# Attention with softmax reciprocals read from the transposed tile, the output product in two halves, and everything behind the scores one step later

## What is computed

```python
scores = scale * np.matmul(q, k.transpose(0, 1, 3, 2))
cum = np.cumsum(np.maximum(s, 0.0), axis=-1)
bias = -(cum[:, :, :, None] - cum[:, :, None, :])
scores = np.where(causal, -1000000000.0, scores + np.minimum(bias, 0.0))
attn = np.exp(scores - np.max(scores, axis=-1, keepdims=True))
attn = attn / (np.sum(attn, axis=-1, keepdims=True) + 1e-09)
attn_out = np.matmul(attn, v)
x = xn(attn_out) ; h = silu(x @ w_gate) * (x @ w_val) ; y = h @ w_out     # xn: RMS norm
h = y @ w_in ; out = (h - np.tanh(h)) @ moe2_w_out
```

## Time and profile before

| what | value |
|---|---|
| three runs, median | 1107.66 us (1103.31 to 1108.92) |
| the profiled execution | 1106.37 us |
| its span, first to last instruction | 1104.6 us |
| mean granted clock of PE | 0.997 |
| busy: PE, DVE, ACT, POOL | 1065.3, 431.2, 421.1, 172.2 us |

### The profile page before, as it was taken

One profiled execution on the slowest core, in us unless ns is written; L12 is line 12 of the kernel. 1 busy time (PEld: TensorE's weight loads), 2 busy tenths in 40 slices (PEclk: granted clock), 3 DMA queues, 4 the chain that ended last, 5 costly groups with the idle time before them and its releaser, 6 DMA issues.

```text
span 1104.6 us, 18165 instructions
## 1 busy us (share of the span) xinstructions
PE 1065.3 (96%) x6516; PEld 980.2 (89%) x6516; DVE 431.2 (39%) x1203; ACT 421.1 (38%) x1030; POOL 172.2 (16%) x184
## 2 busy tenths in 40 slices
PE   5888998899999999999999999999999999999998
PEld 4767777689999999999999999999999999999997
DVE  6656666654432222322322333533223232332322
ACT  5666677663431232222222233533223232322322
POOL 8767777640000000000000000000000000000000
PEclk9999999999999999999999999999999999999999
DMA  6555555322200000000000122210000000000000
GB/s 198 171 167 171 172 172 172 112 75 82 65 1 1 1 0 0 0 0 0 0 0 0 29 77 86 87 30 29 1 1 29 0 28 0 0 28 0 28 0 28
DMA packets 61251, 56.40 MB, mean 51 GB/s; under 512 B 7598, under 2 KB 51630, under 8 KB 61194
## 3 DMA queue, kind: packets, MB, share of 16 engines
q1 hardware_dynamic: 61194, 55.67, 16.5%
HBM read 41.63 MB, written 4.87 MB: 42 GB/s over the span
## 4 chain that ended last, share of the span: by engine, by line
PE 91%; DMA 2%; issue 2%; DVE 2%; POOL 1%; ACT 1%; SPq 0%; DVEq 0%; ACTq 0%; POOLq 0%
PE HP L958 15%; PE HP L960 15%; PE HP L959 15%; PE YP L959 11%; PE YP L960 11%; PE YP L958 11%; PE OP L927 5%; PE TP L911 4%; PE SC L896 3%; PE SC L897 2%; DMA RB<-PT 1%; DMA Qraw<-in_qT 1%; POOL KD L399 1%; DVE PR L675 1%; DVE PT L698 0%
## 5 line engine op out<-in xcount | busy, mean ns | idle before, releaser
L958 PE MATMUL HP<-XS,WA 128*128 128x384 f32 x576 | 194.6, 338 | 0.0
L960 PE MATMUL HP<-XS,WA 128*128 128x384 f32 x576 | 193.0, 335 | 0.0
L959 PE MATMUL HP<-XS,WA 128*128 128x384 f32 x576 | 192.7, 335 | 0.0
L777 DVE TENSOR_TENSOR AC<-AC,HP 128x384 f32<-128x384 f32 (+2 forms) x78 | 40.3, 522 | 293.4 <-PE HP L960 293.4
L828 DVE TENSOR_TENSOR AC<-HP,AC 128x384 f32<-128x384 f32 (+1 forms) x108 | 54.3, 512 | 216.3 <-ACT AC L603 216.3
L603 ACT ACTIVATE AC<-HP 128x384 f32<-128x384 f32 x96 | 47.2, 492 | 215.9 <-PE HP L960 215.4
L958 PEld LDWEIGHTS HP<-XS,WA 128*128 128x128 f32 x576 | 108.2, 188 | 2.6 <-issue 0.2
L959 PEld LDWEIGHTS HP<-XS,WA 128*128 128x128 f32 x576 | 108.2, 188 | 2.4
L911 PE MATMUL TP<-ident,PR 128*128 128x128 f32 (+1 forms) x480 | 86.8, 285 | 23.3 <-issue 16.6
L960 PEld LDWEIGHTS HP<-XS,WA 128*128 128x128 f32 x576 | 108.1, 188 | 0.0
L541 ACT ACTIVATE AC<-HP 128x384 f32<-128x384 f32 x72 | 35.4, 492 | 177.8 <-PE HP L960 177.8
(11 more groups left out here) (105 smaller groups left out, 1979.4 us busy)
## 6 DMA issues: line engine op xcount, KB each, us to landing
X<-in_w SPq DMA_DIRECT2D x52, 256.0 KB, 3.0
Kraw<-in_kT SPq DMA_DIRECT2D x16, 576.0 KB, 4.7
Qraw<-in_qT SPq DMA_DIRECT2D x16, 576.0 KB, 5.7
out_rows<-OS SPq DMA_DIRECT2D x18, 256.0 KB, 2.2
QO<-QA SPq DMA_DIRECT2D x15, 288.0 KB, 3.4
Vt<-in_v SPq DMA_DIRECT2D x16, 256.0 KB, 3.0
WRAW<-in_w SPq DMA_DIRECT2D x16, 256.0 KB, 4.3
RB<-PT SPq DMA_DIRECT2D x128, 32.0 KB, 2.2
```

Of the source, the lines that this page charges most:

```text
L777: dve.tensor_tensor(AC[:, m % 2, cols], AC[:, m % 2, cols], HP[:, 1, cols], ALU.mult).then_inc(prod_done if part is None else prod_part, 1)
L958: pe.matmul(dst, w(0), x(0), start=start, stop=False)
L959: pe.matmul(dst, w(0), x(1), start=False, stop=False)
L960: return pe.matmul(dst, w(1), x(0), start=False, stop=stop)
```

## The change

The transfers to RB go, with RB, its semaphores and `evacuated`. DVE multiplies the output in two instructions of 64 partitions each, one per head, whose second factor is PT[0:64] of that head; for hh = 1 the result and the PSUM operand lie in partitions 64 to 127. A copy into PT waits for the output of three steps before instead of the transfer. The lags grow by one, PR gets a fourth buffer, and the mean square is formed one step later. SP's loads, which were spread over the steps of a pair, are issued pair by pair. Behind the loop, one more set of transposes and values is placed around the first two feed-forward products.

```diff
-T_LAG, V_LAG, O_LAG = 2, 3, 4
-RBS = 3
+T_LAG, V_LAG, O_LAG = 3, 4, 5
-SQ_STEPS, MS_STEP, ROOT_STEP = (0, 1, 2, QB), 8, 2 * QB
+SQ_STEPS, MS_STEP, ROOT_STEP = (0, 1, 2, QB), 9, 2 * QB
...
-        PR = sb("PR", [P, 3, 2, PAD + S], F32)
+        PR = sb("PR", [P, 4, 2, PAD + S], F32)
...
-            def load_rb(n):
-
-                z = q_block(n % QB)[1]
-                wait(sp, o_evac, n - RBS + 1)
-                for hh in range(2):
-                    engine, count = evacuated(n, hh)
-                    sp.wait_ge((evac_act, evac_dve)[engine], count)
-                    sp.dma_start(RB[hh * D:(hh + 1) * D, n % RBS, 0:z], PT[0:D, n % 3, hh, 0:z]
-                                 ).then_inc(rb_in[n % RBS], 16)
...
-            for n in range(ALL):
-                k, u = n // QB, n % QB
+            for k in range(B * PAIRS):
                 at, after = divmod(k + 1, PAIRS), divmod(k + 2, PAIRS)
...
                     wait(sp, scores_done, 2 * QB * k)
                     load_decay(*at)
-                if n >= T_LAG:
-                    load_rb(n - T_LAG)
...
+                if k + 1 < B * PAIRS:
                     sp.wait_ge(q_hi, 2 * (k + 2))
                     load_qo(*at)
...
-                if u == 3 and k + 1 < B * PAIRS:
+                if 0 < k < B * PAIRS - 1:
+                    sp.wait_ge(w_lo, k)
+                    load_weights(*at)
+                if k + 1 < B * PAIRS:
                     wait(sp, pv_done, QB * k)
                     load_v(*at, (k + 1) % 2)
...
-                        if ks[0] == 0 and b * STEPS + n >= 3:
-                            before = b * STEPS + n - 3
-                            dve.wait_ge(rb_in[before % RBS], 2 * 16 * (before // RBS + 1))
+                        if ks[0] == 0:
+                            wait(dve, o_evac, b * STEPS + n - 2)
...
-                dve.wait_ge(rb_in[step % RBS], 2 * 16 * (step // RBS + 1))
-                dve.tensor_tensor(X[:, p, bass.ds((b + turn) * S + q0, z)], OP[:, n % 2, 0:z],
-                                  RB[:, step % RBS, 0:z], ALU.mult).then_inc(o_evac, 1)
+                for hh in range(2):
+                    rows = slice(hh * D, (hh + 1) * D)
+                    last = dve.tensor_tensor(X[rows, p, bass.ds((b + turn) * S + q0, z)], OP[rows, n % 2, 0:z],
+                                             PT[0:D, step % 3, hh, 0:z], ALU.mult)
+                last.then_inc(o_evac, 1)
...
             for hh in range(2):
-                transposes(B, -2, hh)
+                transposes(B, -3, hh)
+            values(B, -4)
             pe.wait_ge(mins_done, 2 * B * STEPS)
             pe.wait_ge(w_lo, B * PAIRS)
             gate(0, 0)
+            for hh in range(2):
+                transposes(B, -2, hh)
             values(B, -3)
+            value(0, 0)
             for hh in range(2):
                 transposes(B, -1, hh)
-            value(0, 0)
             values(B, -2)
             values(B, -1)
```

More of the change, by code:

```diff
@@ L219, in build @@
         eps_done = sem("eps_done"); recip_done = sem("recip_done")
-        pad_done = sem("pad_done"); rb_in = [sem(f"rb_in{i}") for i in range(RBS)]
+        pad_done = sem("pad_done");
         t_done = sem("t_done"); evac_act = sem("evac_act"); evac_dve = sem("evac_dve")
@@ L310, in _ @@
             sp.wait_ge(cum_out, 32)
-            for n in range(ALL):
-                k, u = n // QB, n % QB
+            for k in range(B * PAIRS):
                 at, after = divmod(k + 1, PAIRS), divmod(k + 2, PAIRS)
-                if u == 0 and k + 1 < B * PAIRS:
+                if k + 1 < B * PAIRS:
                     wait(sp, scores_done, 2 * QB * k)
                     load_decay(*at)
-                if n >= T_LAG:
-                    load_rb(n - T_LAG)
-                if u == 1 and k + 1 < B * PAIRS:
+                if k + 2 < B * PAIRS:
+                    if k == 0:
+                        sp.wait_ge(qo_first, 2)
+                        sp.wait_ge(klo_first, 2)
+                        sp.wait_ge(qlo_first, 2)
+                    else:
+                        sp.wait_ge(k_lo, 2 * k)
+                        sp.wait_ge(q_lo, 2 * k)
+                    load_qk(*after, k % 2)
+                if k + 1 < B * PAIRS:
                     sp.wait_ge(q_hi, 2 * (k + 2))
                     load_qo(*at)
[L323 to L331, removed]
-                if u == 3 and k + 1 < B * PAIRS:
+                if 0 < k < B * PAIRS - 1:
+                    sp.wait_ge(w_lo, k)
+                    load_weights(*at)
+                if k + 1 < B * PAIRS:
                     wait(sp, pv_done, QB * k)
                     load_v(*at, (k + 1) % 2)
[L335 to L339, removed]
             for k, (src, _, i, sem_free, count) in enumerate(loads):
@@ L458, in exponential @@
                 _, z, nk, _ = q_block(n % QB)
-                pr = PR[0:z, (b * STEPS + n) % 3, hh, PAD:PAD + nk]
+                pr = PR[0:z, n % 4, hh, PAD:PAD + nk]
                 act.wait_ge(mins_done, b * 2 * STEPS + 2 * n + hh + 1)
@@ L471, in evacuate @@
                         wait(act, pv_done, b * STEPS + n - 2)
-                        if ks[0] == 0 and b * STEPS + n >= 3:
-                            before = b * STEPS + n - 3
-                            act.wait_ge(rb_in[before % RBS], 2 * 16 * (before // RBS + 1))
+                        if ks[0] == 0:
+                            wait(act, o_evac, b * STEPS + n - 2)
                         act.activation(PT[:, (b * STEPS + n) % 3, hh, ks[0] * P:ks[0] * P + w], TP[:, 0, 0:w],
@@ L481, in pad @@
                 act.wait_ge(recip_done, b * STEPS + n + 1)
-                act.activation(PR[0:z, (b * STEPS + n) % 3, :, 0:PAD], RR[0:z, n % 4].rearrange("p (h o) -> p h o", o=1).broadcast_to([z, 2, PAD]), ACT.Copy
+                act.activation(PR[0:z, n % 4, :, 0:PAD], RR[0:z, n % 4].rearrange("p (h o) -> p h o", o=1).broadcast_to([z, 2, PAD]), ACT.Copy
                                ).then_inc(pad_done, 1)
@@ L669, in minima @@
                 dve.wait_ge(scores_done, b * 2 * STEPS + 2 * n + hh + 1)
-                wait(dve, t_done, b * NG + groups_of(n - 3, 1)[-1][0] + 1)
+                wait(dve, t_done, b * NG + groups_of(n - 4, 1)[-1][0] + 1)
                 dve.nop(nofuse=True)
@@ L674, in minima @@
                 end = S - P + z
-                dve.tensor_tensor_reduce(PR[0:z, (b * STEPS + n) % 3, hh, PAD:PAD + nk].rearrange("p (a f) -> p a f", a=halves), sc,
+                dve.tensor_tensor_reduce(PR[0:z, n % 4, hh, PAD:PAD + nk].rearrange("p (a f) -> p a f", a=halves), sc,
                                          mask[0:z, end - nk:end].rearrange("p (a f) -> p a f", a=halves),
```

6 lines of the change are left out of this document (1 added, 5 removed).

## The result

| kernel, series | median us | before, same series | ratio, 95% |
|---|---|---|---|
| changed, first | 1115.45 | 1105.66 | 1.0085, 1.0066 to 1.0104 |
| changed, again | 1115.24 | 1109.65 | 1.0046, 1.0029 to 1.0064 |

The change makes the kernel slower, by 0.85% in the first series and by 0.46% in a later one. The changed kernel took the same time in both; the kernel before varied, here and in two more series (1110.10, 1110.39). The forecast was 1108.5, range 1099 to 1116. The first series lies inside that range, but 2.5 us beyond the 1104 to 1113 that the likeliest case had for itself, and the prediction gave "slower" only 0.19. The profiled execution took 1117.03 us, its span 1115.2, against 1106.37 and 1104.6.

What follows compares the result with a forecast made beforehand. PE bounds the kernel, waiting on DVE in the attention stage. Fourteen periods of 13.85 plus 5.4 give 199.3 against 198.4 (+0.9); with +1.3 at the ends, 1106.37 becomes 1108.6, rounded to 1108.5 us; range 1099 to 1116.

Steps and rivals of the forecast that it cites:

- the likeliest case: The forecast itself for the whole kernel, 1108.5 us, with 1104 to 1113 as its own range; chance 0.53.
- What the transfers cost: Attention stage: DVE's waits for the RB transfers cost 15 us over 14 pair periods, which the change removes.
- Rival 4: Attention stage: transfer waits did not cause the irregular time, so the 15 us stay and 20 are added, 1126; chance 0.03.
- The halves: DVE's output product as two 64-partition instructions: 0.64 us a pair of products, +0.43 per step; bounds 0.42 and 0.64.
- Rival 1: DVE's half products overlap as other DVE instructions do, 6.7 us less over 15 pairs, 1101.9; chance 0.20.
- Places A and B: PE per pair: u=4 scores to u=0's last transposes, 3.81 us (+1.11); u=2 scores to the values, 2.88 (+0.23).
- The root's period keeping its 5.4: Attention pair with the root of the mean square: keeps its 5.4 us, as the root still stops ACT.
- The ends, +1.3 with bounds 0 and 2.7: Before and after the 14 periods: extra PE waits once more each, up to 2 x 1.34, less transposes saved early; +1.3 us.
- rival 3: DVE's half products: each 0.10 us dearer than 0.32, 7.5 us more in all, 1116; chance 0.12.
- Rival 2: Attention stage: the extra step of lag uncouples PE from DVE, period 12.51 or below, 20 us less, 1088.5; chance 0.12.

Runs made afterwards that it cites:

- lag_2_one_product: Changed kernel with the lags of before (2, 3, 4) and the output in one 128-partition product, output not the reference's; 1088.92 us, 0.9798 of before.
- rb_output_last: Kernel before with only DVE's product moved behind the copies at the end of its step, transfers and lags kept; 1089.01 us, 0.9808 of before.
- two_whole: Changed kernel with two 128-partition products in place of the halves, the second into an unread buffer, output not the reference's; 1108.03 us, one run.
- one_product: Changed kernel with the output in one 128-partition product again, using the first head's factor throughout, output not the reference's; 1099.63 us, 0.9899 of before.
- after_again: Changed kernel once more, unedited, beside the kernel before in a later series; 1115.24 us, 1.0046 of before.
- qo_first: Changed kernel with QO's load ahead of those of K and Q for the next pair but one; 1112.50 us, 1.0016 of before.

## Why the prediction came out as it did

**What the transfers cost: right.** I had 15 us. lag_2_one_product is the kernel before without transfers (and with the loads pair by pair, QO behind K and Q). From the first scores of u=2 in pair 1 to those in pair 13 its profile has 149.78 us, before's 167.09: 17.3, of which some 1.8 are before's stretch at the lower clock (0.94 from 60 to 90 us). The medians of that series lie 21.5 us apart, since the kernel before was 4 us slower there than its first profile. Rival 4 is excluded. What I didn't see is that the 15 us needed no halves and no lag: rb_output_last gains as much with the transfers in place.

**The halves: right.** For the pair 0.64 was predicted and 0.60 measured, 0.28 and 0.33, and the reading from the earlier trace rows was the right one: two_whole shows 0.19 for neighbours that begin in the same half. By the Trainium skill ("VectorE: DVE Perf Modes", section "Two Vector instructions with no wait between them") an instruction that begins in another quadrant than the last one is held until the earlier ones have finished. The trace agrees: the pair is busy 0.57, and the next instruction starts 0.03 after it. Rival 1 fell with it, and its sum of 6.7 us was near what two_whole gives: 0.54 a pair, 8 us.

**Places A and B: right.** 3.81 and 2.88 predicted, 3.75 and 2.94 measured; period 13.85 and 13.97. The steady waits that took the place of the irregular ones are at the two places named, 0.99 and 0.56. The split was less good: I priced B by itself at 2.65, and one_product shows 2.52, so the halves cost more and the lag less than the working says.

**The root's period keeping its 5.4: right in the number, in part by luck.** It and the next were to take 2 x 13.85 + 5.4 = 33.1; in after_again they take 17.21 + 15.83 = 33.04. But by my own reading 1.4 of the 5.4 were time at the lower clock, and in after_again there is none: there the root's period has 3.24 over a regular one and the next, which I took for regular, 1.86. The 35.68 of the first profile are these and 2.6 at the lower clock.

**The ends, +1.3 with bounds 0 and 2.7: the step that failed.** They measured -0.14 + 1.41 + 4.54 = 5.8, 4.5 over the term and 3.1 over its upper bound. The text gave QO "most of a pair until it is read". PE shows no wait for it in any pair but the first. There QO is issued at 13.24, behind K and Q, and PE stands from 19.70 to 23.25; this wait of 3.55 us ate what the start should have given back (qo_first). And I counted places A and B once more at the end, but not the drain: a third step of transposes and values is left when the scores are done. From lag_2_one_product to one_product the tail up to the FFN stage grows from 17.26 to 21.02, by the lag alone; the halves add 0.86.

**The miss in sum.** That 1115.45 is inside the range is luck: its upper end, 1116, was the price of rival 3, whose dearer half doesn't exist, and what filled the room was the ends and the clock's stretch, which no rival had. The profiled span grew by 10.6 and not by 2.2. Of the 8.4 between, the ends make 4.5, the twelve periods 12 x 0.12 = 1.4, the clock's stretch 2.6. The median of the later series, on its own kernel before, grew by 5.6.

**Rival 2, that the lag uncouples PE from DVE: wrong here.** Without transfers the longer lag costs 0.34 to 0.63 in each period and 3.6 to 3.8 us in the tail. Place A shows why: PE's own work between two events of DVE got shorter, DVE's did not.

In ratios, what became of the change: transfers gone -2.0%; one more step of lag +1.0% (one_product against lag_2_one_product); halves +1.5% (after_again against one_product). The three come from different series, and the mean clocks differ too: the kernel before had 0.992 beside lag_2_one_product's 0.998. The order of loads makes up 0.3 points of it (qo_first against after_again).

The kernel before varies by 4 us between series while the changed one doesn't, and most of that goes with the clock. In its 45 executions of the three later series the mean granted clock lies between 0.986 and 0.997, on average 0.993; a straight line through them gives 0.8 us for each 0.001 and 1107.2 at 0.997, the clock of its first profile (1106.37). What stays open is why the clock falls more often in those series, and why one execution has the stretch at the lower clock and another not. That the transfers land at other times on other chips fits, but wasn't tried.

## What to carry to other kernels

Before a wait is removed at a price, look at what is queued behind it: here moving the product behind the copies brought 1.9%, and replacing its transfers brought a loss of 0.5 to 0.9%. A longer lag between stages isn't free: list what each engine does between the two events that tie them, at the old lag and the new, and count the drain at the end. Where loads are put in a new order, check the first round by itself.

## What the runs showed of the hardware

A change of halves between neighbouring DVE instructions costs about 0.1 us (0.28 and 0.33 from start to start against 0.19 and 0.20), and the instruction behind is late whether it is a copy or a minimum. Not expected: with no change of halves a second product of 128 x 128 costs no more than 0.19, so doing all of the work twice was cheaper than splitting it (13.43 against 13.97 a period). Nor was it expected that the granted clock of a period was 0.83, with a stretch at 1.2 GHz behind a wait of PE of 1.85 us, in one execution and 1.00, behind the same wait, in another.
